# Step 0's keys in two transfers, a square root two places earlier on ScalarE, and one body of the schedule spread wider with two of its units at its end

## The chip, the cores and the metric

The kernel runs on one core of a Trainium2 chip. The metric is the device time of one launch, in microseconds (us); lower is better. All numbers here come from runs of the kernel before the change and from the profile of one of its executions. In the profile PE is TensorE (PEld its weight loads), DVE is VectorE, ACT is ScalarE, POOL is GpSimd and SP is the queue of SyncE, which issues nearly all transfers.

## What is computed

Three networks in a row, in float32. The first is a delta-rule attention over 4 batches and 8 heads with head dimension 48 and 768 tokens; the other two are feed-forward networks over the 3072 tokens of width 384.

```python
def _attn_ref(q, k, v, beta):
    k_n = k / (np.linalg.norm(k, axis=-1, keepdims=True) + 1e-06)
    state = np.zeros((B, H, D, D))
    for t in range(S):
        kt, vt, bt = k_n[:, :, t], v[:, :, t], beta[:, :, t, None]
        y[:, :, t] = einsum('bhd,bhde->bhe', q[:, :, t], state)
        v_old = einsum('bhde,bhd->bhe', state, kt)
        state = state + bt[:, :, :, None] * einsum('bhd,bhe->bhde', kt, vt - v_old)
...
h = x @ w_in                                        # first network, 384 -> 2048 -> 384
g = where(h >= 1, h, where(h <= -1, 0, (h + 1) ** 2 / 4));  x = g @ w_out
...
xn = x / sqrt(mean(x * x) + 1e-6) * rms_g           # second network, 384 -> 1536 -> 384
y = (silu(xn @ w_gate) * (xn @ w_val)) @ w_out2
```

## The kernel before

**Attention.** The 768 tokens are cut into 6 steps of 128, each step into two halves (`hf` 0 and 1) of 64 tokens. A step's work is written as units, named by kind, step and half. `GK` is the Gram matrix of the keys (keys against keys), `GQ` keys against queries, `Z` and `X` two parts of a triangular inverse, `KS` keys against the state, `U` the updates, `QS` queries against the state, `PU` the output, `KU` the new state. Each is 32 small matmuls in the code (64 rows in the trace, as each float32 matmul is two there). `KU` ends in two DVE additions to `state` (L1262), `PU` of step 1 in two ACT copies to `prob` (L1050). On DVE alone runs the inversion, 31 dependent pairs of operations per step (`inv`, L1167 and L1171), after the square root of the norms on ACT (`nrm`, L1019) and five small operations.

**First network.** Weights and activations are split in a high and a low float32r part, so that each product takes three matmuls. A unit of it (`h0`, `h1`, `h`, `o0`, `o1`, `o`; L1469 and L1487) is three matmuls. The tokens come in tiles: tiles 0 and 1 are the halves of step 0 and are 256 columns wide, the tiles after them are whole steps, 512 wide. Tile 2 holds the output of step 1.

**The schedule.** `PLANS` is one list of units per body, worked out in Python before the kernel is built; every engine walks through the same list in order and picks out its own part, so the order on one engine is the order on all. `first_body` writes body 0 out by hand: it splits the weights (`piece`, `low`, `hi`) while step 0 is inverted. `next_body(k)` gives each attention unit a place as a share of the body's forward units and puts it between them. Body 1 holds tiles 0 and 1, step 1, and the start of step 2; body 2 holds tile 2 and step 2. Nothing moves a unit at run time.

**Between step 1 and tile 2.** `PU` of step 1 leaves its output in `prob`. SP stores it to memory in another order (L873) and, once that has landed, loads it back (L878, `repack`). Then `XE` makes tile 2: ACT writes `xh` (L1061), DVE writes `xl` (L1267). The first matmul of tile 2 waits for `xh`, the third for `xl`. `XE` on ACT also waits for the last `h` of tile 1.

**Banks.** `banks()` gives each attention unit one or two of three PSUM banks in turn, and `banks_free` makes PE wait until what stood there has been evicted. `GQ` of step 2's first half takes a bank that `KU` of step 1's second half used just before it, in the order of units.

**The start.** The keys of step 0 (`kqT[0]`, 48 features of each of two groups of batches, in partitions 0 to 47 and 64 to 111) come in four transfers of 48 partitions, two issued by SP and two by ACT; the source in memory has 128 rows, with zeros in the rest. The first two feed `GK` of half 0, the others `GK` of half 1. PE fills the time with matmuls on the identity matrix (`warm` and `short`, L1496 and L1500), whose results nobody reads.

Of the kernel before, what the change touches and what calls it, by code (L numbers as in the profile page):

```python
# [11 lines left out]
P = 128  # L12
B, H, S, D = 4, 8, 768, 48
# [8 lines left out]
C = 64  # L22
# [78 lines left out]
def first_body():  # L101
# [17 lines left out]
    for e, _ in inversion(0):  # L119
        if e == ("ft", 0, 0):  # L120
            break
        if e[0] == "nrm":
            out += [("hi", 0, 0), ("GR", 0, 0), ("GR", 0, 2), e, ("hi", 0, 1)]
            continue
        out.append(e)
        if e[0] == "inv":
            n = BESIDE * (e[2] + 1) // INV - done
            out += split(n)
            done += n
# [26 lines left out]
def next_body(k, left):  # L156
# [15 lines left out]
    lead, last = (turned, LAST - 0.02) if k == 1 else (at, LAST)  # L172
    us = solve(k) + serial(k)
    if k == 1:
        ev += [((done + 68 + 10 * hf) / total, ("GQ", k, hf)) for hf in range(HALVES)]
    else:
        ev += [(0.04 + 0.05 * hf, ("GQ", k, hf)) for hf in range(HALVES)]
# [130 lines left out]
def build(nc, kq, k, v, beta, w_in, w_out, w_gate, w_val, w_o2, rms_g, y_out, x2d):  # L308
    ctx = ExitStack()
    with ctx:  # L310
# [127 lines left out]
        with psum_one:  # L438
# [106 lines left out]
            def keys_loaded(c):  # L545

                return 16 * (c // 2 + (1 if c % 2 else BP))
# [49 lines left out]
            def first_keys(eng, bp):  # L597

                eng.dma_start(kqT[0][C * bp:C * bp + D, 0, 0:NPAIR, :].rearrange("p i t -> p (i t)"),
                              kq[0, 0, C * bp:C * bp + D, 0:NPAIR * C]).then_inc(s_k0, 16)  # L600
                eng.dma_start(kqT[0][C * bp:C * bp + D, 0, NPAIR:NINST, :].rearrange("p i t -> p (i t)"),
                              kq[0, 0, C * bp:C * bp + D, NPAIR * C:NINST * C]).then_inc(s_kq[0][0], 16)
# [234 lines left out]
            with nc.Block() as block:  # L837
                @block.sync
                def _(sp):
# [47 lines left out]
                    first_keys(sp, 0)  # L887
# [76 lines left out]
                def _(act):  # L964
# [140 lines left out]
                    first_keys(act, 1)  # L1105
# [196 lines left out]
                def _(pe):  # L1302
# [18 lines left out]
                    def attention(u):  # L1321
# [3 lines left out]
                        if kind == "GK":  # L1325
                            if c == 1 and hf == 0:
                                pe.wait_ge(s_gr, NQ)
                            if c == 0 and hf == 0:
                                pe.wait_ge(s_k0, 16 * BP)
                            elif c == 0 or hf == 0:  # L1330
                                pe.wait_ge(s_kq[0][c % 2], keys_loaded(c))
# [160 lines left out]
                    def split(u):  # L1492
                        kind, at, p = u
                        if kind == "warm":
                            for _ in range(p):
                                pe.matmul(acc[2][:, :], ident[:, :], ident[:, :].unsqueeze(1).to_broadcast([P, NQ, P]),  # L1496
                                          start=True, stop=True)
# [65 lines left out]
```

## Time and profile before

| | us |
|---|---|
| median of 3 runs | 1040.0 |
| lowest and highest | 1039.98 and 1040.58 |
| the profiled execution, as timed | 1040.48 |
| its span, first to last instruction | 1038.7 |
| PE busy in the span | 1023.1 |
| DVE busy | 571.2 |
| ACT busy | 446.0 |

The timed value is 1.78 us longer than the span of the same execution. A busy PE is one with a matmul in its array; pauses under about 0.1 us at the change between two kinds of matmuls count as busy or as idle as the modelled ends of the matmuls fall.

### The profile page before, as it was taken

To read this page: it belongs to the slowest core of one execution; us is meant where nothing else is said; L and a number is where in the kernel's file an instruction comes from. 1 tells how busy PE (TensorE), PEld (TensorE's weight loads), DVE (VectorE), ACT (ScalarE), POOL (GpSimd) and SP (SyncE) were. 2 spreads that over 40 slices of the span, in tenths; PEclk is the share of its full clock that TensorE was granted. 3 is DMA by queue.
4 is the path that set the end of the run, shared out by engine and by line. 5 is a ranking of instruction groups with operands and counts; after the bars stand their busy time and mean duration, and the time that the engine had idled before them with its cause. 6 is when DMAs were issued, how large, how long until landed. Compare 5 with 4: busy or idle time off the path is not lost.

```text
span 1038.7 us, 25028 instructions
## 1 busy us (share of the span) xinstructions
PE 1023.1 (98%) x11080; PEld 845.6 (81%) x11080; DVE 571.2 (55%) x1098; ACT 446.0 (43%) x784; POOL 9.9 (1%) x19
## 2 busy tenths in 40 slices
PE   9999989999999999999999999999999999999998
PEld 4598888777777777777888888888888888888886
DVE  6878859778678777943466444234234333333322
ACT  7754645645544544553576442232232232232121
POOL 1000000000000000000000000000000000000000
PEclk9999999999999999999999999999999999999999
DMA  9204024013212402301512220200100100100101
GB/s 327 94 18 169 3 64 160 16 33 108 99 22 76 140 3 52 104 3 33 183 31 63 90 92 1 61 1 20 42 1 31 31 1 1 31 1 1 31 0 31
DMA packets 31211, 58.85 MB, mean 57 GB/s; under 512 B 2752, under 2 KB 21056, under 8 KB 29696
## 3 DMA queue, kind: packets, MB, share of 16 engines
q1 hardware_dynamic: 30656, 56.47, 17.5%
q8 instruction: 87, 1.43, 0.6%
q10 hardware_dynamic: 448, 0.79, 0.3%
q14 instruction: 20, 0.16, 0.0%
HBM read 43.88 MB, written 13.37 MB: 55 GB/s over the span
## 4 chain that ended last, share of the span: by engine, by line
PE 94%; ACT 2%; DVE 2%; issue 1%; DMA 1%; ACTq 0%
PE bank L805 22%; PE hps L1469 20%; PE acc L1487 19%; PE acc L833 11%; PE hps L805 7%; PE hps L833 4%; PE acc L1515 2%; PE bank L1347 1%; PE bank L1376 1%; PE bank L1395 1%; PE bank L1403 1%; PE bank L1421 1%; PE bank L1438 1%; PE bank L1335 1%; PE bank L1365 1%
## 5 line engine op out<-in xcount | busy, mean ns | idle before, releaser
L713 ACT ACTIVATE g<-bank 128x512 f32<-128x512 f32 x72 | 43.1, 599 | 242.1 <-PE bank L805 129.0
L1469 PE MATMUL hps<-xh,w1h 128*128 128x512 f32 (+1 forms) x336 | 127.7, 380 | 2.2 <-DVE g L1279 2.1
L1487 PE MATMUL acc<-g1h,w2h 128*128 128x512 f32 (+1 forms) x336 | 127.1, 378 | 0.4 <-issue 0.4
L1469 PE MATMUL hps<-xl,w1h 128*128 128x512 f32 (+1 forms) x336 | 122.0, 363 | 0.0
L1487 PE MATMUL acc<-g1l,w2h 128*128 128x512 f32 (+1 forms) x336 | 121.9, 363 | 0.0
L1487 PE MATMUL acc<-g1h,w2l 128*128 128x512 f32 (+1 forms) x336 | 121.8, 363 | 0.0
L1469 PE MATMUL hps<-xh,w1l 128*128 128x512 f32 (+1 forms) x336 | 121.8, 362 | 0.0
L1083 ACT ACTIVATE g1h<-g 128x512 fp32r<-128x512 f32 (+1 forms) x112 | 63.9, 571 | 128.2 <-DVE g L1279 113.0
L1074 ACT ACTIVATE g<-hps,half_c 128x512 f32<-128x512 f32 (+1 forms) x112 | 69.5, 621 | 68.7 <-PE hps L1469 67.3
L1287 DVE TENSOR_TENSOR g1l<-g,g1h 128x512 fp32r<-128x512 f32 (+1 forms) x112 | 68.4, 611 | 48.9 <-ACT g1h L1083 48.6
L1279 DVE SCALAR_TENSOR_TENSOR g<-hps,g 128x512 f32<-128x512 f32 (+1 forms) x112 | 68.2, 609 | 40.8 <-ACT g L1077 40.3
L758 DVE TENSOR_TENSOR pr<-g,hps 128x512 f32<-128x512 f32 x36 | 24.8, 688 | 109.4 <-ACT g L713 109.4
L758 DVE TENSOR_TENSOR pr<-g,bank 128x512 f32<-128x512 f32 x36 | 24.7, 686 | 104.2 <-ACT g L713 104.2
L761 DVE TENSOR_TENSOR g1l<-pr,g1h 128x512 fp32r<-128x512 f32 x72 | 49.9, 693 | 51.1 <-ACT g1h L722 51.1
L722 ACT ACTIVATE g1h<-pr 128x512 fp32r<-128x512 f32 x72 | 45.5, 632 | 71.6 <-DVE pr L758 70.1
L1469 PEld LDWEIGHTS hps<-xh,w1h 128*128 128x128 f32 x336 | 63.1, 188 | 15.6 <-DVE g L1279 3.4
L1487 PEld LDWEIGHTS acc<-g1h,w2h 128*128 128x128 f32 x336 | 63.1, 188 | 12.2
L1469 PEld LDWEIGHTS hps<-xl,w1h 128*128 128x128 f32 x336 | 63.1, 188 | 11.6 <-DVE xl L1267 0.4
L1487 PEld LDWEIGHTS acc<-g1l,w2h 128*128 128x128 f32 x336 | 63.1, 188 | 11.0
L833 PE MATMUL acc<-w2h,g1l 128*128 128x384 f32 x213 | 71.6, 336 | 0.0
L833 PE MATMUL acc<-w2h,g1h 128*128 128x384 f32 x213 | 71.6, 336 | 0.0
L833 PE MATMUL acc<-w2l,g1h 128*128 128x384 f32 x213 | 71.5, 336 | 0.0
(238 smaller groups left out, 2026.7 us busy)
## 6 DMA issues: line engine op xcount, KB each, us to landing
kqT<-kq SPq DMA_DIRECT2D x11, 1024.0 KB, 7.1
v_in<-v SPq DMA_DIRECT2D x6, 768.0 KB, 5.3
k_in<-k SPq DMA_DIRECT2D x6, 768.0 KB, 5.3
x2d<-x2s SPq DMA_DIRECT2D x18, 256.0 KB, 5.5
x2t<-x2d SPq DMA_DIRECT2D x6, 768.0 KB, 5.4
y<-y_t SPq DMA_DIRECT2D x44, 96.0 KB, 2.2
x2d<-prob SPq DMA_DIRECT2D x20, 192.0 KB, 2.9
v_in<-x2d SPq DMA_DIRECT2D x10, 384.0 KB, 3.3
```

The source lines that it names most:

```text
L713: act.activation(silu[:, f % 2, :], gps[f % 2][:, :], ACT.Silu).then_inc(e_silu, 1)
L722: act.activation(prh[:, f % 2, :], pr[:, f % 2, :], ACT.Copy).then_inc(e_prh, 1)
L758: dve.tensor_tensor(pr[:, f % 2, :], silu[:, f % 2, :], vps[f % 2][:, :], ALU.mult).then_inc(e_pr, 1)
L761: dve.tensor_tensor(prl[:, f % 2, :], pr[:, f % 2, :], prh[:, f % 2, :].bitcast(F32), ALU.subtract).then_inc(e_prl, 1)
L805: last = pe.matmul(ps[:, :], wt[:, kk, P * f:P * f + P], xx[n % 2][:, kk, :], start=(e == 0), stop=(e == 3 * KD - 1))
L833: last = pe.matmul(yps[j][:, 0:DM], pp[:, f % 2, js], wt[:, f, :], start=(f == 0 and e == 0), stop=(f == NF2 - 1 and e == 2))
L1074: act.activation(g1[:, f % 2, 0:w], hps[f % 2][:, 0:w], ACT.Relu, bias=half_c[:, 0:1], scale=0.5)\
L1083: act.activation(g1h[:, f % 2, 0:WIDTH[n]], g1[:, f % 2, 0:WIDTH[n]], ACT.Copy).then_inc(s_gh, 1)
L1279: dve.scalar_tensor_tensor(out=g1[:, f % 2, 0:w], in0=hps[f % 2][:, 0:w], scalar=1.0, in1=g1[:, f % 2, 0:w], op0=ALU.max, op1=ALU.min).the ...
L1287: dve.tensor_tensor(g1l[:, f % 2, 0:w], g1[:, f % 2, 0:w], g1h[:, f % 2, 0:w].bitcast(F32), ALU.subtract).then_inc(s_gl, 1)
L1469: last = pe.matmul(hps[f % 2][:, 0:WIDTH[n]], wt[:, kk, P * f:P * f + P], xx[:, kk, COLS[n]], start=(kk == 0 and e == 0), stop=(kk == KD - ...
L1487: last = pe.matmul(acc[j][:, 0:WIDTH[n]], wt[:, f, P * j:P * j + P], gg[:, f % 2, 0:WIDTH[n]], start=(f == 0 and e == 0), stop=(f == NF1 - ...
```

## The change

There are four edits. Step 0's keys come in two transfers of all 128 partitions, both from SP. In body 0, ACT takes the root of the norms before two reads of the Gram matrix (`GR`), no longer after them. The second matmul of the first `warm` unit is 256 columns wide, no longer 512. And in `next_body(1)` the places of step 1's units reach to 0.91 of the body instead of 0.89, with the last one, `KU` of half 1, taken out of the row and put at 0.995; in body 2, `GQ` of half 0 stands at the very start, no longer at 0.04.

```diff
         if e[0] == "nrm":
-            out += [("hi", 0, 0), ("GR", 0, 0), ("GR", 0, 2), e, ("hi", 0, 1)]
+            out += [("hi", 0, 0), e, ("GR", 0, 0), ("GR", 0, 2), ("hi", 0, 1)]
             continue
...
-    lead, last = (turned, LAST - 0.02) if k == 1 else (at, LAST)
+    lead, last = (turned, LAST) if k == 1 else (at, LAST)
     us = solve(k) + serial(k)
+    if k == 1:
+        us.remove(("KU", k, HALVES - 1))
+        ev.append((0.995, ("KU", k, HALVES - 1)))
     if k == 1:
         ev += [((done + 68 + 10 * hf) / total, ("GQ", k, hf)) for hf in range(HALVES)]
     else:
-        ev += [(0.04 + 0.05 * hf, ("GQ", k, hf)) for hf in range(HALVES)]
+        ev += [((0.09 * hf if k == 2 else 0.04 + 0.05 * hf), ("GQ", k, hf)) for hf in range(HALVES)]
...
             def keys_loaded(c):
-                return 16 * (c // 2 + (1 if c % 2 else BP))
+                return 16 * (c // 2 + 1)
...
-            def first_keys(eng, bp):
-
-                eng.dma_start(kqT[0][C * bp:C * bp + D, 0, 0:NPAIR, :].rearrange("p i t -> p (i t)"),
-                              kq[0, 0, C * bp:C * bp + D, 0:NPAIR * C]).then_inc(s_k0, 16)
-                eng.dma_start(kqT[0][C * bp:C * bp + D, 0, NPAIR:NINST, :].rearrange("p i t -> p (i t)"),
-                              kq[0, 0, C * bp:C * bp + D, NPAIR * C:NINST * C]).then_inc(s_kq[0][0], 16)
+            def first_keys(eng):
+
+                eng.dma_start(kqT[0][:, 0, 0:NPAIR, :].rearrange("p i t -> p (i t)"), kq[0, 0, :, 0:NPAIR * C]).then_inc(s_k0, 16)
+                eng.dma_start(kqT[0][:, 0, NPAIR:NINST, :].rearrange("p i t -> p (i t)"),
+                              kq[0, 0, :, NPAIR * C:NINST * C]).then_inc(s_kq[0][0], 16)
...
-                    first_keys(sp, 0)
+                    first_keys(sp)
...
-                    first_keys(act, 1)
...
-                            for _ in range(p):
-                                pe.matmul(acc[2][:, :], ident[:, :], ident[:, :].unsqueeze(1).to_broadcast([P, NQ, P]),
+                            for n in range(p):
+                                w = NQH if p < NQ and n else NQ
+                                pe.matmul(acc[2][:, 0:w * P], ident[:, :], ident[:, :].unsqueeze(1).to_broadcast([P, w, P]),
```

**The border of bodies 1 and 2 on PE.** The names are those of the trace: `L1487` (after the change `L1488`) are units `o`, `L1469` (`L1470`) units `h`; matmuls of 256 columns are tile 1, of 512 tile 2. Before:

```order
L1487 MATMUL acc<-g1l,w2h 128x256
L1469 MATMUL hps<-xh,w1h 128x512
L1469 MATMUL hps<-xh,w1l 128x512
L1469 MATMUL hps<-xl,w1h 128x512
L1469 MATMUL hps<-xh,w1h 128x512
L1469 MATMUL hps<-xh,w1l 128x512
```

After the change, at the same place, with the semaphores that PE waits for:

```order
L1488 MATMUL acc<-g1l,w2h 128x256
L1439 MATMUL bank<-upd,k_in 48x48 [waits upd_ready,attn_y_ready]
L1439 MATMUL bank<-upd,k_in 48x48 x31
L1348 MATMUL bank<-kqT 64x64 [waits q_turned_loaded0,state_ready,attn_y_ready]
L1348 MATMUL bank<-kqT 64x64 x31
L1470 MATMUL hps<-xh,w1h 128x512 [waits g_ready,xh_ready]
L1470 MATMUL hps<-xh,w1l 128x512
```

`KU` of step 1 (L1439) and `GQ` of step 2 (L1348) now stand between the last unit of tile 1 in this body and the first unit of tile 2, and `GQ` waits for `state_ready`, which DVE raises when it has added `KU`'s first bank to `state`.

**The border on DVE.** `xl` is the low part of tile 2, `outer` and `inv` the inversion of step 2, `g` the activation of tile 1, `state` the two additions of `KU`. Before, `KU`'s additions are 22 rows above `xl`, and this stands at the border:

```order
L1287 TENSOR_TENSOR g1l<-g,g1h 128x256
L1267 TENSOR_TENSOR xl<-v_in,xh 128x512 x3
L1167 TENSOR_TENSOR outer<-sysm,inv 128x231
L1171 TENSOR_TENSOR inv<-inv,outer 128x21x11
L1279 SCALAR_TENSOR_TENSOR g<-hps,g 128x256
```

After the change:

```order
L1288 TENSOR_TENSOR g1l<-g,g1h 128x256
L1268 TENSOR_TENSOR xl<-v_in,xh 128x512 x3
L1168 TENSOR_TENSOR outer<-sysm,inv 128x220
L1172 TENSOR_TENSOR inv<-inv,outer 128x22x10
L1280 SCALAR_TENSOR_TENSOR g<-hps,g 128x256
L1263 TENSOR_TENSOR state<-state,bank 128x384 x2
```

The additions to `state` have come to stand behind `xl`, one pair of the inversion and one `g`.

**The dense stretch of body 1 on PE.** From `GK` of step 2 on (L1335, after the change L1336), with the units of the first network between. Before:

```order
L1335 MATMUL bank<-kqT 64x64 x32
L1487 MATMUL acc<-g1h,w2h 128x256
L1487 MATMUL acc<-g1h,w2l 128x256
L1487 MATMUL acc<-g1l,w2h 128x256
L1487 MATMUL acc<-g1h,w2h 128x256
L1487 MATMUL acc<-g1h,w2l 128x256
L1487 MATMUL acc<-g1l,w2h 128x256
L1335 MATMUL bank<-kqT 64x64 x32
```

Between the same two there are three forward units after the change instead of two. In forward units from the start of the body, the places are, before and after: `GK` 135 and 137, 137 and 140; `KS`, `U`, `QS`, `PU`, `KU` of half 0 at 140, 142, 145, 148, 150 and 143, 146, 149, 152, 155; of half 1 at 153, 155, 158, 160, 163 and 158, 160, 163, 166, 186. `XE` stands at 182 in both. In bodies 3 to 5 nothing has moved.

## Rows read from the trace of the kernel before

**Rows 1.** The page: span, and busy time of each engine (share, instructions).

```profile
span 1038.7 us, 25028 instructions
...
PE 1023.1 (98%) x11080; PEld 845.6 (81%) x11080; DVE 571.2 (55%) x1098; ACT 446.0 (43%) x784; POOL 9.9 (1%) x19
```

**Rows 2.** Windows of body 1: length, busy us (instructions) by engine, PEclk, DMA share, GB/s.

```profile
100.00:110.00 10.00, 10.00 (x84) 9.79 (x82) 9.66 (x27) 5.63 (x15) 0.00 (x0) 1.00 0.01 2
...
120.00:130.00 10.00, 8.51 (x283) 7.61 (x282) 9.19 (x17) 5.78 (x15) 0.00 (x0) 1.00 0.02 3
130.00:140.00 10.00, 8.49 (x288) 7.50 (x286) 3.43 (x11) 4.23 (x11) 0.00 (x0) 1.00 0.19 42
140.00:150.00 10.00, 8.74 (x282) 7.67 (x283) 4.39 (x14) 3.46 (x8) 0.00 (x0) 1.00 0.16 45
```

**Rows 3.** PE's timeline, 120 to 150 us: start, us, what, [idle before <-releaser].

```profile
132.16 0.67 PE L1403 MATMUL bank<-kqT,state 48*48 48x64 f32 x33 [0.80 <-issue]
...
138.89 1.15 PE L1376 MATMUL bank<-state,kqT 48*64 48x48 f32 x64 [0.71 <-DVE state L1262]
...
145.52 0.43 PE L1403 MATMUL bank<-kqT,state 48*48 48x64 f32 x12 [0.87 <-issue]
```

**Rows 4.** DMA queues, 143.0 to 144.4 us: packets, MB, share of 16 engines.

```profile
q8 instruction: 1, 0.02, 4.6%
```

**Rows 5.** Timeline of the first 12 us, PE and ACT.

```profile
1.61 3.65 PE L1496 MATMUL acc<-ident 128*128 128x512 f32 x4 [1.61 <-POOL ident L941]
...
5.19 1.16 PE L1335 MATMUL bank<-kqT 48*64 48x64 f32 x64
...
7.06 1.16 PE L1335 MATMUL hps<-kqT 48*64 48x64 f32 x64 [0.70 <-DMA kqT<-kq]
8.15 3.70 PE L1496 MATMUL acc<-ident 128*128 128x512 f32 x8
...
11.84 0.26 ACT L1019 ACTIVATE nrm<-sysm 128x32 f32<-128x32 f32 x1 [0.19 <-DVE sysm L1133]
```

**Rows 6.** Windows for the DMA share and GB/s, the last two columns.

```profile
2.40:3.30 0.90, 0.90 (x2) 0.34 (x1) 0.00 (x0) 0.56 (x1) 0.90 (x3) 1.00 0.88 310
3.30:6.20 2.90, 2.90 (x67) 1.35 (x65) 0.00 (x0) 0.60 (x3) 2.52 (x5) 1.00 1.04 198
...
78.00:88.00 10.00, 8.53 (x65) 7.69 (x64) 7.89 (x21) 3.88 (x10) 0.00 (x0) 1.00 1.01 423
```

**Rows 7.** Timelines from step 1's last `PU` to tile 2; SPq rows are issues.

```profile
146.78 1.11 PE L1421 MATMUL bank<-prob,upd 64*48 64x64 f32 x64
...
158.62 0.40 PE L1469 MATMUL hps<-xh,w1h 128*128 128x512 f32 x1
...
150.36 1.02 DVE L1262 TENSOR_TENSOR state<-state,bank 128x384 f32<-128x384 f32 x2 [2.00 <-PE bank L1438]
...
156.69 0.42 DVE L1279 SCALAR_TENSOR_TENSOR g<-hps,g 128x256 f32<-128x256 f32 x1
157.02 0.37 DVE L1167 TENSOR_TENSOR outer<-sysm,inv 128x220 f32<-128x220 f32 x1
...
158.47 1.90 DVE L1267 TENSOR_TENSOR xl<-v_in,xh 128x512 fp32r<-128x512 f32 x3 [0.32 <-ACT xh L1061]
...
147.96 1.09 ACT L1050 ACTIVATE prob<-bank 128x512 f32<-128x512 f32 x2 [0.50 <-PE bank L1421]
...
157.81 1.68 ACT L1061 ACTIVATE xh<-v_in 128x512 fp32r<-128x512 f32 x3 [0.25 <-PE hps L1469]
...
152.56 0.38 SPq L878 DMA_DIRECT2D v_in<-x2d  x1
```

**Rows 8.** DMA issues, 152 to 153 us: count, KB, us to landing.

```profile
v_in<-x2d SPq DMA_DIRECT2D x1, 384.0 KB, 3.2
```

**Rows 9.** The end: PE's last matmuls, and a window 2 us later (PEclk third from last).

```profile
1032.80 0.69 PE L827 MATMUL acc<-w2h,g1l 128*128 128x384 f32 x3
...
1035.00:1036.00 1.00, 0.00 (x0) 0.00 (x0) 0.00 (x0) 0.00 (x0) 0.00 (x0) 0.91 0.96 260
```

More of the change, by code:

```diff
@@ L1328, in attention @@
                             if c == 0 and hf == 0:
-                                pe.wait_ge(s_k0, 16 * BP)
+                                pe.wait_ge(s_k0, 16)
                             elif c == 0 or hf == 0:
```

## The prediction

> **What bounds the kernel now.** I read the page first. PE is busy for 1023.1 of 1038.7 us [rows 1], so the kernel is a stream of matmuls, and only two things can change its time: matmuls added or taken away, and PE's pauses. The change takes away half of one matmul at the very start, so nearly everything rests on the pauses. I then cut body 1 into windows [rows 2]. From 100 to 110 us PE never stops: 84 matmuls of 256 columns in 10 us, 0.119 us each, so a forward unit (three) takes 0.36 us. In the three windows from 120 to 150 us it is idle for 1.49 + 1.51 + 1.26 = 4.3 us. This is where the units of step 1 stand close together. Last I read PE's own timeline there, to see what ended each pause, and the three engines' timelines at the border of bodies 1 and 2.
>
> The pauses of the dense stretch are of two kinds [rows 3]. Some end with another engine: 0.71 us before `KS` of half 1, for the additions to `state` on DVE. Others end with "issue", no engine at all, and two of them lie inside a `QS`, between two of its own matmuls: 0.80 us before 132.16 and 0.87 us before 145.52. No data can be late there. One block of instructions was fetched between 143.0 and 144.4 us [rows 4], just before PE stopped. I take these pauses as PE's instructions arriving late: an attention unit is 64 matmuls in 1.1 us, a forward unit three in 0.36 us, so a dense row of attention units eats instructions several times as fast.
>
> **Wider units in body 1.** The units from `GK` of step 2 to `PU` of half 1 had 25 forward units among them (135 to 160) and get 29 (137 to 166), while `KU` leaves. The pause for `state` should go almost whole: the root of step 2's norms now stands ahead of `PU`, so DVE is no longer held behind it when `KU` ends, and I count 0.6 of 0.71 us. The remaining pauses sum to 4.3 - 0.7 = 3.6 us. Of these 1.67 us are the two inside `QS`. A third forward unit puts 0.36 us more between two bursts, against 0.80 and 0.87: that takes away a little under half. I use the same half for all of the 3.6 us, 1.8 us. Together -2.4 us. The bounds are -1.0 (only the pauses for data shrink, and the fetch has the same block borders inside bursts) and -4.3 us, all of it.
>
> **Two units at the border.** This decides the case. In the trace before, `PU` of half 1 ends at 146.78 + 1.11 = 147.9 us and tile 2 begins on PE at 158.62 [rows 7], 10.7 us later. Under it runs the repacking: ACT copies `prob` until 149.05; the load back is issued at 152.56 and lands 3.2 us later [rows 8], at 155.8, that is 7.9 us after `PU`. ACT begins `xh` only at 157.81, released by the last `h`, so the repacking had 2 us to spare. It costs nothing today.
>
> After the change `PU` stands at 166 and the last `h` of tile 1 is the 183rd unit. From the end of `PU` to the end of that `h` PE has 17 units, 17 x 0.36 + 0.1 = 6.2 us. The repacking still takes 7.9 us. So `xh` begins at 8.0 us after `PU`, and now the transfer releases it. PE meanwhile does three units `o` (to 7.3 us) and `KU` (0.95 us, to 8.3 us) and comes to `GQ`, which needs the bank that `KU` has just filled. What evicts it stands on DVE behind `xl`, a pair of the inversion and a `g`. From the rows: `xl` begins 158.47 - 157.81 = 0.66 us after `xh` and takes 1.90 us, ending 10.56 us after `PU`; the pair takes 0.37 + 0.37 (10.6 to 11.3), `g` about 0.35 more (its 0.42 us less the overlap of 0.09 with the next row), to 11.65; the first of the two additions half of 1.02 us, to 12.15. `GQ` can begin at 12.2 us. PE has been idle since 8.3: a new pause of 3.9 us. Behind the waiting `GQ` are all matmuls of tile 2, so nothing fills it. The first of them starts at 12.2 + 1.1 = 13.3 us, by when `xl` is long there; the 0.1 us that PE waited for `xl` at 158.9 goes. I count +3.8 us. The lower bound does not depend on the repacking: were it early, `xh` would begin 0.25 us after the last `h`, at 6.45 us, and `GQ` at 10.65, still a pause of 2.3 us. The upper bound is 4.5 us, with a transfer 0.6 us longer. `GQ` cannot go ahead of DVE's list, and DVE has no spare path: the order is fixed.
>
> **The clock after a pause of that length.** At the end of the kernel PE's last matmul ends at 1032.80 + 0.69 = 1033.5 us, and in the window from 1035 to 1036 the granted clock averages 0.91 [rows 9]. With half speed as the lower level, it fell for the last 0.18 us of that window, at 1035.8, 2.3 us after PE stopped. The longest pause in the body so far was 0.9 us, with the clock at 1.00. A pause of 3.9 us is longer than 2.3, so I expect it to fall to 1.2 GHz before PE resumes. How long it stays there is bounded by the start: the two 512-column matmuls from 1.61 us take 3.65 us, 1.83 each, against 3.70 for four, 0.92 each, at 8.15; and `GK` at 5.19 is already as fast (1.16 us) as at 7.06 [rows 5]. So the slow stretch at the start was at most 3.6 us long (1.61 to 5.19). Work at half speed for 2.0 to 3.6 us loses 1.0 to 1.8 us; I take +1.4. The Trainium skill, in "TensorE: Matmul & The Clock Gate", section "Why this matters for your kernels", warns of idle gaps between bursts of matmuls for the same reason; by that page this term belongs in the sum, while by the rows of the body alone, where no pause has cost any clock, the sum would be 1.4 us less.
>
> **The start.** PE's work from 8 us on hangs on the second keys (`GK` at 7.06 us waited 0.70 us for them). Four times 48 rows of 4 KB are 0.79 MB; twice 128 rows are 1.05 MB, 0.26 MB more. With transfers from both queues under way the DMA engines moved 198 GB/s from 3.30 to 6.20 us, against 423 GB/s for large transfers from SP alone between 78 and 88 us [rows 6]. If the slow rate stays, 0.26 MB cost 0.26 / 0.198 = +1.3 us. If it came from the two queues and goes, the 0.57 MB of that time take 1.36 us and the rest 0.62: 2.0 instead of 2.9 us, -0.9. The rate was already 310 GB/s before 3.30 us with both queues in use, so neither is excluded, and I take 0. The Trainium skill, in "DMA: Bandwidth & Descriptors", section "Issuing engines are not separate DMA queues", says that transfers from different engines interleave on the same 16 DMA engines, and that issuing from several saves sequencer time only. By it the queues explain no slow rate and the bytes alone count, +0.6 to +1.3 us; no row here isolates this.
>
> The root of the norms at 11.84 us waited for DVE's transposes (0.19 us, [rows 5]) and not for the two reads ahead of it, so moving it brings 0. The reads now come behind it and end about 0.7 us later, into ACT's time before the first `low`; 0 as well. The shorter `warm` ends at 4.4 instead of 5.3 us, and `GK` has to wait for its keys anyway: 0, with a risk below.
>
> **Sum.** -2.4 + 3.8 + 1.4 + 0 = +2.8 us. The profiled execution took 1040.48 us, 0.5 more than the median, so 1043.3 against it and 1042.8 against the median of 1040.0. Its own range is 1041.3 to 1044.2 us (dense stretch and clock to either side).
>
> **The rivals.** *The clock holds.* The pause is there but PE resumes at full speed. For it: one fall, at the end, is thin evidence. Against it: 3.9 is well over 2.3. -2.4 + 3.8 = +1.4: 1041.4 us.
>
> *The dense stretch gives nearly all it has.* If the instructions are only just too slow now, the wider row frees all 4.3 us. For it: the pauses are all under 0.9 us. Against it: `U` of half 1 still has only two forward units ahead of it. -4.3 + 3.8 = -0.5 without a fall of the clock: 1039.5 us, not slower. It decides as soon as the stretch gives more than 3.8 us, and with early keys (-0.9) it would be 1038.6.
>
> *The clock rises late at the start.* PE now idles between the shorter `warm` and `GK`. If the clock then stays low for up to 3.6 us more, the second `GK` (1.16 us) and part of the four `warm` matmuls take twice their time: +1.8 us over the forecast, 1044.6. For it: before, PE worked without a break until the clock was up. Against it: it still works through most of that time.
>
> **How the numbers follow.** About 0.2%, 2.1 us, is what a measurement of this kernel can tell from no change. Chances: forecast 0.48, the clock holds 0.27, the stretch gives all 0.13, late clock at the start 0.12. Slower by over 2.1 us are three quarters of the forecast (0.36), the late clock (0.11) and a little of the second (0.03): 0.50. Faster by over 2.1 us is only the end of the third case with early keys: 0.07. The rest, 0.43, is within. For 8 in 10 the range runs from 1039.0 to 1044.7 us.
>
> **What would show it.** PE's row of `GQ` at the border has an idle time of about 3.9 us, ended by DVE's `state`; ACT's `xh` is released by the transfer and no longer by PE; the granted clock falls below 1.00 near 159 us and the first matmuls of tile 2 take twice their time. Windows over the dense stretch show about 2 us of idle time instead of 4.3. `GK` of half 1 stands at 7.06 us, within -0.9 and +1.3. The forecast is wrong if PE does not wait at `GQ`, which only an eviction ahead of `xl` could bring, or if the dense stretch gives over 4 us.

## The result: 5.9 us slower

The changed kernel took 1045.88 us in the median of 7 runs (1043.28 to 1047.11), the kernel before 1039.98 us on the same chip (1039.61 to 1041.07, 7 runs). The ratio is 1.0051, with a 95% interval of 1.0042 to 1.0060. The forecast was 1042.8 us with a range of 1039.0 to 1044.7: the direction was right and the median lies outside the range. The profiled execution took 1046.47 us; its span is 1044.7 us, 6.0 more than before.

The page of the changed kernel, its span and the busy times, against [rows 1]:

```profile
span 1044.7 us, 25026 instructions
PE 1027.1 (98%) x11080; PEld 849.5 (81%) x11080; DVE 571.8 (55%) x1098; ACT 446.1 (43%) x784; POOL 10.1 (1%) x19
```

PE is busy for 4.0 us more, though half a matmul was taken away. So it did not only wait longer, it also worked more slowly somewhere. Its timeline at the border of bodies 1 and 2, in place of the PE rows of [rows 7]:

```profile
148.97 1.11 PE L1422 MATMUL bank<-prob,upd 64*48 64x64 f32 x64
...
157.40 0.94 PE L1439 MATMUL bank<-upd,k_in 64*48 64x48 f32 x64
162.66 1.99 PE L1348 MATMUL bank<-kqT 48*64 48x64 f32 x64 [4.32 <-issue]
164.58 0.79 PE L1470 MATMUL hps<-xh,w1h 128*128 128x512 f32 x1
...
178.70 0.39 PE L1470 MATMUL hps<-xh,w1h 128*128 128x512 f32 x1
```

`GQ` (L1348) stands after 4.32 us of idle time and then takes 1.99 us where the same work took 1.16; the first `h0` of tile 2 takes 0.79 instead of 0.40 us. The pause is put down to "issue", since the instruction that held PE waits for several semaphores and none is named; what it waited for is read from ACT and DVE in the same place:

```profile
158.49 1.67 ACT L1063 ACTIVATE xh<-v_in 128x512 fp32r<-128x512 f32 x3 [2.39 <-DMA v_in<-x2d]
...
159.15 1.89 DVE L1268 TENSOR_TENSOR xl<-v_in,xh 128x512 fp32r<-128x512 f32 x3 [2.48 <-ACT xh L1063]
160.97 0.38 DVE L1168 TENSOR_TENSOR outer<-sysm,inv 128x220 f32<-128x220 f32 x1
161.38 0.39 DVE L1172 TENSOR_TENSOR inv<-inv,outer 128x220 f32<-128x220 f32 x1
161.68 0.42 DVE L1280 SCALAR_TENSOR_TENSOR g<-hps,g 128x256 f32<-128x256 f32 x1
162.02 1.00 DVE L1263 TENSOR_TENSOR state<-state,bank 128x384 f32<-128x384 f32 x2
```

`xh` is released by the load and no longer by PE; then come `xl`, the pair, `g` and the two additions to `state`. The first addition ends half of 1.00 us after 162.02, at 162.5, and `GQ` starts at 162.66. This is the chain of the prediction, row by row. Windows over the same stretch show the clock (PEclk is third from last):

```profile
158.40:162.60 4.20, 0.00 (x0) 0.00 (x0) 3.41 (x8) 2.86 (x6) 0.00 (x0) 0.81 0.15 20
162.70:168.00 5.30, 5.30 (x72) 4.49 (x73) 4.22 (x10) 0.00 (x0) 0.00 (x0) 0.51 0.34 135
168.00:178.00 10.00, 10.00 (x111) 8.36 (x110) 7.91 (x17) 5.78 (x11) 0.00 (x0) 1.00 0.42 124
```

The trace's record of the granted clock has the fall at 161.04 us, 2.7 us after PE stopped, and the rise back at 167.86: PE runs at 1.2 GHz and not at 2.4 from the end of the pause until then.

At the start PE reads, against [rows 5]:

```profile
1.61 2.93 PE L1498 MATMUL acc<-ident 128*128 128x512 f32 x4 [1.61 <-POOL ident L943]
4.71 1.99 PE L1336 MATMUL bank<-kqT 48*64 48x64 f32 x64 [0.17 <-DMA kqT<-kq]
6.47 1.93 PE L1336 MATMUL hps<-kqT 48*64 48x64 f32 x64
8.33 4.93 PE L1498 MATMUL acc<-ident 128*128 128x512 f32 x8
```

Both `GK` start about half a microsecond sooner than before (5.19 and 7.06), as their keys are there sooner; but both take 1.9 to 2.0 us instead of 1.16, and `warm` 4.93 instead of 3.70. The clock rose only at 10.85 us, before the change at 4.99.

To divide the 6.0 us I take three places that both traces have on PE: the first matmul of tile 1 (50.43 us before, 51.04 after), the 31st `h` matmul of 512 columns, in tile 2 (172.68 and 178.70), and the end of the span. From the third to the end there are 866.0 us in both. So 0.6 us arise before tile 1, nothing behind 180 us, and the stretch between, "tile 1 to tile 2" below, grows from 122.25 to 127.66 us, by 5.4.

### The profile page after: what moved, and what is told of

Read it like the earlier page. It is cut to its first block, busy times and chain, and to the rows that moved or that the text cites. A ratio compares the mean times of both kernels' runs of the same rounds, so it can differ in the third digit from the quotient of the medians.

```text
span 1044.7 us, 25026 instructions
## 1 busy us (share of the span) xinstructions
PE 1027.1 (98%) x11080; PEld 849.5 (81%) x11080; DVE 571.8 (55%) x1098; ACT 446.1 (43%) x784; POOL 10.1 (1%) x19
## 4 chain that ended last, share of the span: by engine, by line
PE 95%; ACT 1%; DVE 1%; issue 1%; DMA 0%; ACTq 0%
PE bank L807 21%; PE hps L1470 20%; PE acc L1488 20%; PE acc L835 10%; PE hps L807 7%; PE hps L835 4%; PE acc L1517 2%; PE bank L1348 1%; PE bank L1377 1%; PE bank L1396 1%; PE bank L1336 1%; PE bank L1404 1%; PE bank L1439 1%; PE bank L1422 1%; PE bank L1366 1%
## 5 line engine op out<-in xcount | busy, mean ns | idle before, releaser
L1470 PE MATMUL hps<-xh,w1h 128*128 128x512 f32 (+1 forms) x336 | 128.5, 382 | 2.2 <-DVE g L1280 2.1
L1488 PE MATMUL acc<-g1h,w2h 128*128 128x512 f32 (+1 forms) x336 | 127.0, 378 | 0.0
L1470 PE MATMUL hps<-xh,w1l 128*128 128x512 f32 (+1 forms) x336 | 122.5, 365 | 0.0
L1470 PE MATMUL hps<-xl,w1h 128*128 128x512 f32 (+1 forms) x336 | 122.2, 364 | 0.0
L1488 PE MATMUL acc<-g1h,w2l 128*128 128x512 f32 (+1 forms) x336 | 122.0, 363 | 0.0
L1488 PE MATMUL acc<-g1l,w2h 128*128 128x512 f32 (+1 forms) x336 | 121.7, 362 | 0.0
L1470 PEld LDWEIGHTS hps<-xh,w1h 128*128 128x128 f32 x336 | 63.5, 189 | 16.0 <-DVE g L1280 3.4
L1488 PEld LDWEIGHTS acc<-g1h,w2h 128*128 128x128 f32 x336 | 63.1, 188 | 12.2
L1470 PEld LDWEIGHTS hps<-xl,w1h 128*128 128x128 f32 x336 | 63.5, 189 | 11.3 <-DVE xl L1272 0.2
L1488 PEld LDWEIGHTS acc<-g1l,w2h 128*128 128x128 f32 x336 | 63.1, 188 | 11.0
```

The source lines that it names most:

```text
L1470: last = pe.matmul(hps[f % 2][:, 0:WIDTH[n]], wt[:, kk, P * f:P * f + P], xx[:, kk, COLS[n]], start=(kk == 0 and e == 0), stop=(kk == KD - ...
L1488: last = pe.matmul(acc[j][:, 0:WIDTH[n]], wt[:, f, P * j:P * j + P], gg[:, f % 2, 0:WIDTH[n]], start=(f == 0 and e == 0), stop=(f == NF1 - ...
```

## The experiments

All change the kernel before, unless said otherwise, and were timed in the same rounds as it; its median in the four groups was 1039.63, 1040.25, 1039.64 and 1040.12 us. "Over before" is worked out as (ratio - 1) x 1040 us.

### The schedule and the start apart

**e1, the schedule alone:** the edits in `next_body`, nothing at the start.

```diff
-    lead, last = (turned, LAST - 0.02) if k == 1 else (at, LAST)
+    lead, last = (turned, LAST) if k == 1 else (at, LAST)
+        us.remove(("KU", k, HALVES - 1))
+        ev.append((0.995, ("KU", k, HALVES - 1)))
-        ev += [(0.04 + 0.05 * hf, ("GQ", k, hf)) for hf in range(HALVES)]
+        ev += [((0.09 * hf if k == 2 else 0.04 + 0.05 * hf), ("GQ", k, hf)) for hf in range(HALVES)]
```

> The kernel before with the edits of the schedule alone (the wider row of step 1, `KU` of half 1 at 0.995, `GQ` of step 2 at 0); keys, `warm` and root as before. Theory now, read from the trace after: dense stretch -1.4, pause ahead of `GQ` 4.3, half clock behind it +2.2, so +5.1 us, 1045.1 us. By the sizes of the prediction it would be +2.8, 1042.8 us. Rival: the late clock at the start carries the miss, and this kernel lies near 1042.

Measured 1045.09 us, ratio 1.0054 (1.0041 to 1.0066). The stretch from tile 1 to tile 2 takes 127.54 us, and PE's row is that of the changed kernel:

```profile
161.25 1.99 PE L1350 MATMUL bank<-kqT 48*64 48x64 f32 x64 [4.47 <-issue]
```

The schedule alone carries nearly all of the loss.

**e2, the start alone:** keys, shorter `warm` and root as changed, the schedule of before.

> The three edits of the start alone (keys in two transfers, second `warm` matmul halved, root sooner), with the schedule of before in bodies 1 and 2. Theory now: the clock rises near 10.9 us and no longer at 5.0, the first split matmul stands 1.4 us later, 0.9 of it reaches tile 1, the rest is given back in body 0: 1040.9 us. The prediction's forecast for this part: 1040.0. Its rival of the late clock: 1041.8.

Measured 1039.75 us, ratio 1.0003 (0.9994 to 1.0012): no difference. In this execution the clock rose at 4.71 us, and tile 1 began at 49.01 us, sooner than in any other profile here. So the same edits gave 0.6 us more in the changed kernel's profile and 1.4 less in this one, with the clock's rise as the visible difference.

**e16, the changed kernel once more,** on another chip.

> The changed kernel once more, on this chip. Theory: the pause at `GQ` is 4.3 to 4.5 us again, and the clock falls just behind its end each time, for 2.3 us lost or 1.5 if the half clock is as short as with the whole `warm`; the clock's rise at the start falls anywhere between 4.7 and 12.8 us. Rival: where the clock rises early this kernel comes to 1043.3 and where late to 1047.

Measured 1045.50 us, ratio 1.0058 (1.0045 to 1.0071), runs from 1045.0 to 1048.5. This time the clock rose at 5.80 us, tile 1 began at 49.22, and yet the kernel was no faster, so the rival is wrong. The pause at `GQ` was longer, not the same as before as the theory had it:

```profile
161.68 1.99 PE L1348 MATMUL bank<-kqT 48*64 48x64 f32 x64 [5.05 <-issue]
```

SP's issues explain it. From the store of `prob` to the load back, which waits for the store to land:

```profile
149.55 0.82 SPq L875 DMA_DIRECT2D x2d<-prob  x2
154.25 0.38 SPq L880 DMA_DIRECT2D v_in<-x2d  x1
```

That is 4.70 us; in the first profile of the changed kernel it was 4.02 (151.26 to 155.28), and the pause was 4.32. The transfer took 0.68 us longer and the pause 0.73. In the kernel before it was 3.49 us, the second shortest of the eighteen profiles (3.45 in e10, up to 5.08 in e9); there it is hidden, here every part of it is seen.

**e8, the shorter `warm` alone.**

```diff
-                            for _ in range(p):
-                                pe.matmul(acc[2][:, :], ident[:, :], ident[:, :].unsqueeze(1).to_broadcast([P, NQ, P]),
+                            for n in range(p):
+                                w = NQH if p < NQ and n else NQ
+                                pe.matmul(acc[2][:, 0:w * P], ident[:, :], ident[:, :].unsqueeze(1).to_broadcast([P, w, P]),
```

> The kernel before with the second matmul of the first `warm` halved, and nothing else. Theory: PE idles between `warm` and `GK`, and in some executions the clock rises near 11 and not near 5 us, which costs 2.0 us there: a wider spread than that of the kernel before, median 0 to 2 us above it. Rival: the late rise in the trace after came from the keys or was chance that hits the kernel before as well: 1039.6 with its spread.

Measured 1040.62 us, ratio 1.0004 (0.9995 to 1.0013), runs from 1039.6 to 1042.6, those of the kernel before from 1039.1 to 1042.4. In the profiled execution, its slowest, the clock rose at 12.76 us:

```profile
5.18 1.99 PE L1335 MATMUL bank<-kqT 48*64 48x64 f32 x64 [0.65 <-DMA kqT<-kq]
7.01 1.99 PE L1335 MATMUL hps<-kqT 48*64 48x64 f32 x64
8.93 5.59 PE L1497 MATMUL acc<-ident 128*128 128x512 f32 x8
```

Tile 1 began at 52.53 us. Of the four profiles with the shorter `warm` (changed kernel twice, e2, e8) two have the rise at 10.85 and 12.76 us and two at 4.71 and 5.80. The fourteen with the whole one have it between 4.59 and 7.79 us. So the late rise very probably belongs to the shorter `warm`, though two cases are few; it does not come every time, and the median shows no loss beyond what these runs resolve.

**e9, the keys alone,** in two transfers of 128 rows.

> The kernel before with step 0's keys in two transfers of 128 rows, `warm` and root as before. Theory: both halves of the keys are there by 6.2 us and `GK` of half 1 follows `GK` of half 0 without a wait, 0.8 us earlier at tile 1: 1038.8 us. Rival: what follows hangs on DVE and on the other transfers, which start no earlier: 1039.6.

Measured 1040.70 us, ratio 1.0000 (0.9991 to 1.0009): nothing, and my theory of 0.8 us is wrong. `GK` of half 0 starts at 5.32 us, when `warm` ends, and that of half 1 follows at 6.64 without a wait for its keys; e1, with four transfers, has 5.32 and 6.67. The keys do not set the time here as soon as `warm` lasts this long.

**e3, the changed kernel with the first `warm` whole.**

> The changed kernel with the first `warm` whole again (two matmuls of 512 columns), everything else as changed. Theory: the short `warm` is what lets the clock rise late in some executions; with the whole one it rises near 4.7 to 6.2 us, and what is left is the border and the dense stretch: 5.2 us over the kernel before, with a narrower spread than the changed kernel (1043.3 to 1047.1). Rival: the start carries nothing, and this one lies 5.9 us over the kernel before, as the changed kernel does.

Measured 1045.59 us, ratio 1.0057 (1.0044 to 1.0069), spread 1045.2 to 1046.5. The spread is narrower as expected, the median is that of the changed kernel: restoring `warm` wins nothing that can be measured. The clock rose at 4.59 us and tile 1 began at 49.45. But from the 31st `h` matmul of 512 columns to the end this profile has 867.0 us and not 866.0: 1.0 us was lost at the next border. The store of step 2 took 4.96 us from issue to the load back there, and 3.43 to 4.08 in the fifteen profiles other than e3, e6 and e11. Those two have 5.05 and 5.00 us, and lose 1.3 and 1.0 us at the same place. In e11:

```profile
245.48 1.67 ACT L1064 ACTIVATE xh<-v_in 128x512 fp32r<-128x512 f32 x3 [1.48 <-DMA v_in<-x2d]
...
255.02 1.16 PE L1356 MATMUL bank<-kqT 48*64 48x64 f32 x64 [0.75 <-DVE prob L1251]
```

`xh` of tile 3 is late, DVE with it, and `GQ` of step 3 waits for its eviction.

### The border

**e4, the wider row alone:** `LAST` as changed, `KU` five units behind `PU`, no unit at the border.

```diff
-    lead, last = (turned, LAST - 0.02) if k == 1 else (at, LAST)
+    lead, last = (turned, LAST) if k == 1 else (at, LAST)
+        us.remove(("KU", k, HALVES - 1))
+        ev.append((0.915, ("KU", k, HALVES - 1)))
```

> The kernel before with the wider row alone: `KU` of half 1 leaves the row but stands five units behind `PU` (0.915), `GQ` of step 2 stays at 0.04. Theory now: only the pause for `state` and some of the pauses put down to issue go, -1.4 us, 1038.6 us. The prediction's size: -2.4, 1037.6. Rival: the row gives nothing by itself, and what the trace after shows less of pauses there was the missing `KU`: 1039.5 or more.

Measured 1040.14 us, ratio 1.0006 (0.9997 to 1.0014): no gain, against my theory. The reason is at the border:

```profile
157.95 0.50 PE L1472 MATMUL hps<-xh,w1h 128*128 128x512 f32 x1 [1.05 <-ACT xh L1064]
```

In the dense stretch PE is idle for 2.7 of the 30 us from 120 to 150 us, before for 4.3. But `PU` stands six units later (2.2 us), the repacking has lost its 2 us to spare, and PE waits 1.05 us for `xh`. The stretch from tile 1 to tile 2 takes 122.30 us, before 122.25. The wider row shortens one pause and opens another of nearly the same size.

**e5, `KU` at the border, `GQ` four units into tile 2.**

> The kernel before with the wider row and `KU` of half 1 at 0.995, but `GQ` of step 2 at 0.04 as before, so that four units of tile 2 stand between them. Theory: PE then waits only for `xh` and `xl` (0.9 us) and perhaps 0.3 us at `GQ`, too short for the clock to fall; with -1.4 of the row 1039.8 us. Rival: the late transfer and the late `KU` cost nearly as much by themselves, about 1043.

Measured 1041.98 us, ratio 1.0022 (1.0013 to 1.0031), so 2.3 us over before. The profile has the two waits of the theory, 0.70 us for `xh` and 0.52 at `GQ`, and a stretch of 123.48 us:

```profile
157.67 0.50 PE L1472 MATMUL hps<-xh,w1h 128*128 128x512 f32 x1 [0.70 <-ACT xh L1064]
...
161.17 1.16 PE L1350 MATMUL bank<-kqT 48*64 48x64 f32 x64 [0.52 <-issue]
```

`GQ` takes 1.16 us: after 0.70 us of idle time the clock has not fallen. So what makes the border expensive is not `KU` there but `GQ` behind it. The profiled execution took 1040.78 us, the slowest 1044.5; what stands in the slower ones I cannot say.

**e7, `GQ` first in body 2 with `KU` early** (0.915).

> The wider row with `KU` of half 1 five units behind `PU` (0.915), and `GQ` of step 2 at the very start of body 2. Its bank is then evicted long before, so `GQ` (1.1 us) runs in the pause of 1.05 us that the wide row alone showed ahead of `xh`. Theory: 1.05 us less than the wide row alone (1040.1), so 1039.1 us. Rival: `GQ` waits for something else at the border and the pause stays: 1040.1.

Measured 1041.54 us, ratio 1.0009 (1.0000 to 1.0018): not faster, against the theory. The pause ahead of `xh` is gone, as expected, and the stretch is no shorter (122.64 us), because another has come 14 us on:

```profile
172.07 0.50 PE L1472 MATMUL hps<-xh,w1h 128*128 128x512 f32 x1 [0.98 <-DVE g L1282]
```

DVE is no slower: from `xl` to this `g` it takes 12.62 us here (158.72 to 171.34) and 12.61 in e4 (157.93 to 170.54). But PE has `GQ` behind it already, comes to the matmul that needs this `g` about 1 us sooner, and waits there. The work moved forward is given back as soon as DVE sets the pace.

**e6 and e11, the pause filled:** the schedule edits alone, with matmuls on the identity matrix ahead of `GQ`, into the bank that is free. They add work whose result nobody reads.

```diff
+                        if u == ("GQ", 2, 0):
+                            v, j = BANKS[u][0][1]
+                            pe.wait_ge(evicted[v[0]], evictions(v, j))
+                            for _ in range(8):
+                                pe.matmul(bank_of(u, 0)[:, :], ident[:, :], ident[:, :].unsqueeze(1).to_broadcast([P, NQ, P]),
+                                          start=True, stop=True)
```

> The schedule edits alone (as in the first experiment), with eight matmuls of 512 columns on the identity matrix written to the free bank ahead of `GQ` of step 2, 8 x 0.46 = 3.7 us, inside the pause of 4.5. Theory: `GQ` starts when it started, but the clock does not fall, so that 2.2 us come back: 1042.9 us. Rival: the half clock is not caused by the pause, or what follows waits for another engine anyway: 1045.1.

Measured 1047.21 us, ratio 1.0061 (1.0047 to 1.0074). I had taken a row's 0.46 us for a matmul, but a matmul in the code is two rows: the eight took 7.13 us and ran past the pause by 2.7. They do keep the clock at 2.4 GHz. With four:

> The schedule edits alone with four matmuls of 512 columns on the identity matrix ahead of `GQ` of step 2. The eight of the earlier run took 7.13 us, 0.89 each, and so ran past the pause; four take 3.6 us of the 4.5. Theory: `GQ` starts when it started in the first experiment, at full clock, and 2.3 us come back: 3.1 us over the kernel before instead of 5.4. Rival: nothing comes back, 5.4 over.

```profile
155.90 3.70 PE L1330 MATMUL bank<-ident 128*128 128x512 f32 x8
160.42 1.16 PE L1356 MATMUL bank<-kqT 48*64 48x64 f32 x64 [0.82 <-issue]
...
174.16 0.39 PE L1478 MATMUL hps<-xh,w1h 128*128 128x512 f32 x1
```

`GQ` still waits for `state`, 0.82 us, and then takes 1.16 and not 1.99 us. From its start to the 31st matmul of 512 columns there are 174.16 - 160.42 = 13.74 us, in the changed kernel 178.70 - 162.66 = 16.04. The same matmuls take 2.3 us longer behind the pause of 4.3: that is the price of the clock. In the other kernels with this border the same stretch took 16.10 (e1), 15.74 (e16) and 15.25 us (e3), so the price ran from 1.5 to 2.4 us. The median was 1044.32 us, ratio 1.0043 (1.0031 to 1.0056), 4.5 us over before and not 3.1 as expected; the profiled execution, the fastest, was at 1042.96. So the clock term is shown in the traces, while the medians of e1 and e11 (1.0054 and 1.0043, intervals overlapping, and the two timed in different groups) do not prove it; why e11's median lies 1.4 us above its own profile is open.

### The dense stretch

**e12, the row's end left where it was** and only `KU` taken out of it, so that `PU` stands at 163.

> The kernel before with `KU` of half 1 taken out of the row (at 0.915) and the row's end left at 0.89, so that `PU` of half 1 stands at unit 163 instead of 160 (166 in the wide row). Theory: the pause of 1.05 us ahead of `xh`, which ate the gain of the wide row alone, goes, since three units (1.1 us) more lie between `PU` and tile 2, and about 0.7 us of the dense stretch's pauses is kept: 0.7 us below the kernel before. Rival: the pauses put down to issue only move, no gain.

Measured 1041.33 us, ratio 1.0016 (1.0007 to 1.0025): slower, against the theory. PE waited 0.56 us for `xh` and 0.54 for `xl` (the transfer took 4.50 us here), and two pauses in the row were as long as ever:

```profile
132.84 0.76 PE L1406 MATMUL bank<-kqT,state 48*48 48x64 f32 x36 [1.17 <-issue]
...
146.07 0.49 PE L1406 MATMUL bank<-kqT,state 48*48 48x64 f32 x18 [0.98 <-issue]
```

**Where the pauses stand.** In the changed kernel:

```profile
133.25 0.88 PE L1404 MATMUL bank<-kqT,state 48*48 48x64 f32 x45 [0.31 <-issue]
...
141.35 0.38 PE L1377 MATMUL bank<-state,kqT 48*64 48x48 f32 x10 [0.54 <-issue]
...
147.13 0.65 PE L1404 MATMUL bank<-kqT,state 48*48 48x64 f32 x27 [1.04 <-issue]
```

A group's count says how many rows were left after the pause: 45 of `QS` of half 0, 10 of `KS` and 27 of `QS` of half 1. Count what the trace has of PE before each pause, weight loads, matmuls and semaphore instructions: these three pauses stand at instructions 4800, 5314 and 5568. The two inside `QS` of the kernel before [rows 3] stand at 4802 and 5568, though each lies elsewhere in its unit. All five lie 192 to 194 above a multiple of 256. (The expectation of e10 below gives 4614 and 5374 for the two: that count leaves the semaphore instructions out and lies 188 and 194 lower.) A block of instructions fetched is one packet of 0.02 MB, as in this view of the queues of the changed kernel from 144.0 to 146.2 us, just ahead of the pause at 147.13:

```profile
q8 instruction: 1, 0.02, 2.9%
```

It started at 144.69 us and PE went on 2.44 us later; for the other pauses this is 2.2 to 2.7 us. The Trainium skill, in "Advanced Engine Details and Errata", section "ISA Cache", gives 16 KB and 256 instructions as one line of the instruction cache; the places of the pauses here agree with that. What a late block costs, the profiles show: 0.26 to 1.42 us (e10 and e9). The cost changes from execution to execution: in the nine profiles with the wider row and its end at 0.91 (changed kernel twice, e1, e3 to e7, e11) the pause at 4800 lasts 0.30 to 0.86 us and the one at 5568 lasts 0.76 to 1.04.

**e10, the blocks' borders moved** by 128 instructions: 32 more `short` matmuls at the start.

> The kernel before with 32 more `short` matmuls at the start (0.12 us each in the trace's rows of two, 128 more instructions on PE). Theory: the pauses inside `QS` stand at every 256th instruction of PE (in the trace before after row 31 of half 0 and row 52 of half 1, instructions 4614 and 5374 by my count), so 128 instructions more move them: none at those two rows any more, and new ones near row 37 of `U` of half 0, row 19 of `PU` of half 0, row 4 of `KS` of half 1, and ahead of `QS` of half 1. Rival: they belong to `QS` (its operands or its place) and stay at rows 31 and 52. Time: 32 matmuls x 0.25 = up to 8 us more at the start, of which body 0 may give some back; it is not what is asked.

Both pauses inside `QS` are gone, each `QS` is one group of 64 rows:

```profile
138.05 1.11 PE L1403 MATMUL bank<-kqT,state 48*48 48x64 f32 x64
...
149.47 0.31 PE L1395 MATMUL bank<-v_in,tt 64*64 64x48 f32 x2 [0.26 <-issue]
150.97 1.11 PE L1403 MATMUL bank<-kqT,state 48*48 48x64 f32 x64
```

One new pause stands two rows before the end of `U` of half 1, at instruction 5571, which is 195 above a multiple of 256 like the others; with 128 instructions added ahead, that is a place 128 instructions earlier in the program than before. It is 0.26 us long. The stretch from tile 1 to tile 2 takes 120.92 us, 1.3 less than before, with no unit of it moved. The kernel as a whole is 6.9 us slower (1046.51), since the added matmuls take 7.2 us at the start.

**e13, e14, e15: the same shift at little cost,** with small matmuls in place of one large `warm`.

```diff
-    out = [("warm", 0, 2), ("GK", 0, 0), ("GK", 0, 1), ("warm", 0, 4), ("short", 0, 6)]
+    out = [("warm", 0, 2), ("GK", 0, 0), ("GK", 0, 1), ("warm", 0, 3), ("tiny", 0, 32), ("short", 0, 6)]
```

> The kernel before with 32 small matmuls (64x64x64 on the identity matrix, 128 instructions, 1.1 us by `GK`'s row) in place of the last 512-column matmul of the second `warm` (0.9 us). Theory: PE's instructions come in blocks of 256 and a pause stands at a block's border when too few microseconds of work lie ahead of it; 128 more instructions ahead move the borders to where 32 more `short` did (1.3 us less between tile 1's first matmul and tile 2), here at nearly no cost: 1.3 - 0.2 = 1.1 us under the kernel before. Rival: the gain in that run came from the start being later, everything behind it better filled: no gain.

> The same with 16 small matmuls (64 instructions). Theory: the borders move by 32 rows of an attention unit: from row 52 to about row 21 of `QS` of half 1, from row 31 of `QS` of half 0 out of it, one to about row 36 of `KS` of half 1 (which waits for `state` just ahead, so its instructions are there). A pause stays in `QS` of half 1 at row 21, the one in `QS` of half 0 goes: 0.4 to 0.8 us gained, less than with 128. Rival: `QS` of half 1 pauses at row 52 as before.

> The 32 small matmuls together with step 0's keys in two transfers and the root sooner, the first `warm` whole and the schedule of before: all that showed no cost. Theory: 1.1 us under the kernel before from the borders, and 0 to 0.4 from the start (keys alone measured 0.0): 1.3 us under it. Rival: 0.

| | median | ratio | interval | tile 1 to tile 2 |
|---|---|---|---|---|
| e13, 128 instructions | 1040.30 | 1.0000 | 0.9991 to 1.0008 | 121.74 |
| e14, 64 instructions | 1040.76 | 1.0004 | 0.9995 to 1.0013 | 121.19 |
| e15, 128 with keys and root | 1039.84 | 0.9997 | 0.9988 to 1.0006 | 121.66 |

None is faster. All three lack the pauses inside `QS`, also at row 21 where I expected one in e14; PE is idle for 2.8 to 3.3 of the 30 us from 120 to 150 us, where it was idle for 4.3. But the stretch as a whole shrinks by only 0.5 to 1.1 us, and the median by nothing: the borders have moved everywhere, also into units that had none. The same shift of 128 instructions gave 1.3 us in e10 and 0.5 and 0.6 in e13 and e15, so the size of this gain is known to no better than that. In e14 a border now cuts `KU` of step 0:

```profile
53.89 0.30 PE L1438 MATMUL bank<-upd,k_in 64*48 64x48 f32 x7 [0.67 <-issue]
```

No version of mine is measurably faster than the kernel before.

## Why the forecast was 3 us too low

**The border pause: mechanism right, size 0.4 short.** Forecast 3.9 us of idle time and +3.8; it was 4.32, and 4.47, 4.52 and 5.05 in e1, e3 and e16. Every step of the chain held: `KU` ended 8.3 us after `PU` (158.34 - 150.08), `xh` began 8.4 us after it (8.0 forecast), the rest followed by the durations of [rows 7]. The 0.4 us are the landing of the store, for which I had one number, and nearly the luckiest: 3.49 us. A wait on a transfer wants the spread of that transfer in its range; mine, 0.6 us to the upper side, still left out e16 and touched e3.

**The clock: mechanism right, +1.4 forecast, +2.3 measured.** That it would fall was right, and the rival of the clock that holds is wrong in all four profiles that have this pause. The reason given, "3.9 us is longer than 2.3", was weaker than it looked: the 2.3 us at the end of the kernel before is one value of a wide spread, 2.2 to 5.2 us over the eighteen profiles. At the border the fall came 2.7, 3.0, 4.6 and 2.8 us after PE stopped (changed kernel, e1, e3, e16), in e3 only when `GQ` had already begun (161.60 against 161.52 us). So there was some luck in it. The step that failed is the bound of its length, "the slow stretch at the start was at most 3.6 us long". The half clock of the start says nothing of the one after a fall in the body: from the end of the pause to the rise it was 5.2 us (162.66 to 167.86), and all of that was matmuls at half speed. In e3, where it was 3.4 us, the loss was 1.5, inside the forecast's 1.0 to 1.8; in e1 and e16 it was 2.4 and 2.0.

**The dense stretch: -2.4 forecast, about -1.2 measured.** The stretch from tile 1 to tile 2 grew by 5.4 us, of which 4.3 are the pause and 2.3 the clock; what is left is -1.2. The pause for `state` did go, for all of its 0.71 us. The step that failed is the one that gave half of each pause put down to issue to the third forward unit. The cause I had named, instructions arriving late, was right; but such a pause stands at a fixed step of 256 instructions, not between two bursts. Another forward unit shifts which rows stand there, and does not take the border away. One pause in `QS` went from 0.87 to 1.04, the other from 0.80 to 0.31, and a new one of 0.54 opened in `KS`. These sizes are chance in part: the same place as the 0.31 took 0.57, 0.85 and 0.56 us in e1, e3 and e16. The gain as a whole varies with them. Taken as the time from tile 1 to the end of `KU` plus the 13.74 us of e11 behind it, against 122.25, it is -1.2 in the changed kernel, -1.5, -1.0, -0.9, -0.6 and -1.1 in e1, e3, e5, e6 and e16, and -2.3 in e11. One of seven reached the forecast. What sets the size of one such pause stays open. And the wider row was costed as if it stood alone: e4 shows that its gain, such as it is, was already owed to `xh` through the later `PU`.

**The start: 0 forecast, +0.6 in the profile, 0.1 to 0.4 in the medians.** The rival of the late clock came true in two of four profiles of the shorter `warm`. I gave it 0.12, which was too little, but its price in the median is small: what lies behind it in body 0 gives some back (the first split matmul stood 1.4 us later in the changed kernel, tile 1 0.6). The keys came out as forecast, 0 (e9), though by another way: in the changed kernel's profile both `GK` start 0.5 and 0.6 us sooner, and the median of e9 shows no gain. The Trainium skill, in "DMA: Bandwidth & Descriptors", section "Rules for kernel authors", advises one transfer of 128 partitions instead of two of half the partitions; this trace agrees in so far as it lost nothing by the extra 0.26 MB. The root was never tested alone; in e2 and e15 it costs nothing that shows.

**The sum** of the profile: 0.6 + 4.3 + 2.3 - 1.2 = 6.0 us. The forecast had 0 + 3.8 + 1.4 - 2.4 = 2.8. All four terms erred to the same side, and the range, made by spreading each a little, did not reach them.

What stays open is the spread of the kernels with a border wait. The changed kernel ran from 1043.3 to 1047.1 us and e11 from 1043.0 to 1045.6, two times or more the spread of the kernel before on the chips concerned; e3, with the same border, kept within 1.3 us in five runs. The landing of the store is one source at this border and, in e3, e6 and e11, at the next; the length of the half clock (1.5 to 2.4 us of loss) is another. Whether they are all, one profile per kernel cannot tell.

## What to carry to other kernels

A wait that today is covered by a few microseconds of slack is priced by that slack: before later work is moved past it, count what both the moved unit and the lengthened row take from the same slack, since in e4 the lengthened row used it up by itself. When PE idles for a few microseconds, add the price of the clock to the pause; here it was a third to a half as much again (1.5 on 4.5 in e3, 2.3 on 4.3 in the changed kernel). Matmuls that nobody needs can give back that price at most and never the pause. Pauses that end with "issue" inside a unit of small matmuls belonged to instruction fetch here: find them by instruction number and not by what stands around them, and expect any change of the count ahead of them to move all of them, for better here and worse there.

## What the runs showed of the hardware

The clock also fell after a pause far shorter than that of the border. In e2 PE's longest wait ahead of the fall was 0.65 us, and the granted clock was at half from 113.94 to 120.77 us; in e9 from 115.30 to 118.72, after a wait of 0.61 us. These are windows of e2:

```profile
105.00:113.90 8.90, 8.17 (x180) 7.40 (x178) 7.88 (x14) 3.74 (x10) 1.10 (x1) 1.00 0.01 3
114.00:120.70 6.70, 6.70 (x148) 6.12 (x149) 3.29 (x9) 4.89 (x14) 0.00 (x0) 0.50 0.02 5
```

The same waits stand there in the kernel before with the clock at 1.00, so this comes in some executions only. It cost about 1.2 us (a stretch from tile 1 to tile 2 of 123.43 in e2 and 123.54 in e9, against 122.25 us). The Trainium skill, in "TensorE: Matmul & The Clock Gate", section "Why this matters for your kernels", warns of idle gaps of some microseconds between bursts; the border's pause is such a one and the trace agrees; the falls of e2 and e9 came after waits well under a microsecond. The stretch at half clock behind the border's pause was 6.8 us long in the changed kernel, in its repetition and in e1, counted from the fall, and 3.4 us in e3.

How soon the clock falls once PE stops for good differs as widely: behind PE's last matmul of the kernel it took from 2.2 us (the changed kernel) to 5.2 us (its repetition, the same program).
